# Later sums for the down product's last operands, and six attention pairs in other slots

## The chip, the core and the metric

The kernel runs on one core of a Trainium2 chip. The engines that compute are TensorE (PE), VectorE (DVE), ScalarE (ACT) and GpSimd (POOL); SyncE (SP) issues nearly all the DMAs. They run their own instruction streams and meet at semaphores. The metric is the device time of the one launch in microseconds.

## What is computed

Attention over keys and values that are averaged in groups of eight, and behind it two feed-forward layers over the 4608 resulting rows (the attention output with heads side by side), cut to its core:

```python
k_p = k.reshape(B, H, Sp, pool, D).mean(axis=3)      # B, H, S, D = 8, 8, 576, 64; pool = 8
v_p = v.reshape(B, H, Sp, pool, D).mean(axis=3)
scores = scale * np.matmul(q, k_p.transpose(0, 1, 3, 2))
attn = np.exp(scores - scores.max(-1)); attn = attn / (attn.sum(-1) + 1e-09)
x = np.matmul(attn, v_p)                             # as rows of 512
...
h = x @ w_in;  r = np.maximum(h, 0.0);  x = (s * (r * r) + b) @ w_out      # 512 -> 2048 -> 512
...
h = x @ w_in2; g = h * (1.0 / (1.0 + np.exp(-h)));  return g @ w_out2
```

## The kernel before, in words

**Units and phases.** The first 576 rows are worked in a first stage with plain products. The other 4032 rows form six units, two halves each: the widths of a half are `HALVES = (288, 288, 360, 360, 360, 360)`. The first two are the narrow units, the other four the wide ones. A unit has two phases, an even one for the first layer and an odd one for the second; there are twelve, `ph` 0 to 11. A phase has 56 slots, one granule of weights each (a row of `w_dram`, 512 KB, in a ring of six places), and 12 matmuls of 288 or 360 columns. Slots 0 to 27 are the up product, in four groups `g` of seven products `j` (a Strassen-like scheme: seven products of sums of quadrants in place of eight). Slots 28 to 55 are the down product; its slot `d` is 0 to 27, its operands stand in `DOWN` as (product j, half h), two slots each, so operand `idx` is used in d = 2 idx and 2 idx + 1: (0,0), (1,0), (0,1), (1,1), (2,0), (2,1), (3,0), (3,1), (4,0), (4,1), (5,0), (5,1), (6,0), (6,1).

**How an operand is made.** Every operand is a quadrant of the hidden layer `gq` or a difference of two. `combine(ph, j, h)` on DVE writes the difference in place (L1269), ACT writes the rounded high part (`dhi`, into `sp_hi`), DVE the rest (`dlo`, L1282 in even phases for some operands, L1285 otherwise, into `sp_lo`), in the loop `down_slot`, with `dhi` and `dlo` of operand idx + 3 in slot d = 2 idx + 1. `combined` counts the sums in the order of `COMBOS`. `form` adds a product that has ended in PSUM to its quadrant (L1244, L1246).

**x of the next unit.** In odd phases, `load_x` on SP brings the next unit's input from `xa_dram` (L512) into the last quadrant of `gq`, which must be free by then: it waits for `dlo` of operand 7. SP reaches it in its slot 28 + RING + 10, between two ring loads, and `load_gran` for slot n waits until PE has done slot n - 6. SP works in order, so what stands behind a waiting instruction waits too. DVE and ACT make x's operands from it in the slots `XR_SLOTS` of the odd phase (`x_slot`: xlo, L1290, and xsum, L1306); in even phases they make those of the second layer from `yb` near the end.

**Attention.** 32 pairs of heads, one `t` each, are spread over the slots by a table written by hand: `UNIT_TURNS` has for each unit the base slots of its pairs and the offsets of 13 turns, `TURN_NAMES`: scores, sub, exp, sum, norm, turn0, lo0, turn1, lo1, values0, add0, values1, add1. A unit's slots count from 0 to 111 over both phases. scores, turn0/1 (transposes) and values0/1 are PE's (L650, L664, L677); sub, sum, norm, lo0/1 and add0/1 are DVE's (L1147, L1152 to L1157, L1160, L1166, L1172); exp and the copies are ACT's; POOL averages keys and values. All of a slot's attention turns stand on each engine ahead of the slot's other work. All use one PSUM tile `t_ps`: turn0 waits for norm, turn1 for lo0, values1 for add0, the scores of the next pair for add1. `sub` of a pair writes `probs`, whose storage holds the last pair's output, so it waits until that has been stored to `xa_dram`; SP issues the store in the slot of add1 plus 7.

## Time and profile before

| | before |
|---|---|
| median of 3 runs | 1683.53 us (1678.99 to 1684.2) |
| profiled execution | 1683.26 us, span 1681.5 us |
| PE busy | 1601.1 us, 95% |
| DVE, ACT, POOL busy | 62%, 54%, 14% |
| mean granted clock of PE | 0.985 |
| DMA | 483.82 MB, 288 GB/s on average |
| chain that ended last | PE 73%, DVE 10%, DMA 9%, ACT 4% |

The span runs from the first to the last instruction; the device time is 1.8 us longer. A busy share says how full an engine is over the whole, not what holds the kernel in a stage: for that one reads a stretch at a time, and in it which wait of PE ends last, who ended it, and what that engine did before.

### The profile page before, as it was taken

To read this page: it belongs to the slowest core of one execution; us is meant where nothing else is said; L and a number is where in the kernel's file an instruction comes from. 1 tells how busy PE (TensorE), PEld (TensorE's weight loads), DVE (VectorE), ACT (ScalarE), POOL (GpSimd) and SP (SyncE) were. 2 spreads that over 40 slices of the span, in tenths; PEclk is the share of its full clock that TensorE was granted. 3 is DMA by queue.
4 is the path that set the end of the run, shared out by engine and by line. 5 is a ranking of instruction groups with operands and counts; after the bars stand their busy time and mean duration, and the time that the engine had idled before them with its cause. 6 is when DMAs were issued, how large, how long until landed. Compare 5 with 4: busy or idle time off the path is not lost.

```text
span 1681.5 us, 26389 instructions
## 1 busy us (share of the span) xinstructions
PE 1601.1 (95%) x10582; PEld 1583.9 (94%) x10582; DVE 1049.7 (62%) x1201; ACT 904.7 (54%) x1156; POOL 237.5 (14%) x294
## 2 busy tenths in 40 slices
PE   7999998888899889899999999999999999999998
PEld 6999897888899879899999999999999999999998
DVE  6787785565574664664765855756747656537454
ACT  4675654634545535547545557455466455474442
POOL 5310120121120221211201101102012010000000
PEclk9999999999999999999999999999999999999999
DMA  5899898887989878898888998888888888988886
GB/s 194 309 347 359 342 372 335 291 261 262 299 304 337 288 255 275 267 355 273 281 262 262 311 304 264 274 269 270 309 295 277 264 262 260 336 267 270 265 266 219
DMA packets 138008, 483.82 MB, mean 288 GB/s; under 512 B 14752, under 2 KB 14752, under 8 KB 135840
## 3 DMA queue, kind: packets, MB, share of 16 engines
q1 hardware_dynamic: 134080, 472.70, 83.0%
q10 hardware_dynamic: 3808, 9.44, 1.4%
q8 instruction: 85, 1.39, 0.3%
q14 instruction: 35, 0.29, 0.1%
HBM read 405.67 MB, written 76.41 MB: 287 GB/s over the span
## 4 chain that ended last, share of the span: by engine, by line
PE 73%; DVE 10%; DMA 9%; ACT 4%; issue 3%; SPq 0%; DVEq 0%; ACTq 0%
PE a_ps L806 19%; PE a_ps L784 18%; PE b_ps L806 14%; PE b_ps L784 13%; DMA xa_dram<-probs 5%; PE a_ps L710 2%; DMA w_raw<-weights 2%; PE t_ps L664 2%; PE t_ps L677 2%; DMA ring<-w_dram 2%; DVE w_sum L1200 1%; DVE gq L1269 1%; PE t_ps L650 1%; DVE sp_lo L1285 1%; DVE probs L1147 1%
## 5 line engine op out<-in xcount | busy, mean ns | idle before, releaser
L784 PE MATMUL a_ps<-xc_hi,ring 128*128 128x360 f32 (+1 forms) x1536 | 390.1, 323 | 16.4 <-DVE gq L1244 8.3
L806 PE MATMUL a_ps<-sp_hi,ring 128*128 128x360 f32 (+1 forms) x1536 | 375.0, 323 | 5.3 <-DMA ring<-w_dram 5.3
L784 PE MATMUL b_ps<-xc_hi,ring 128*128 128x360 f32 (+1 forms) x1152 | 290.6, 318 | 4.2 <-DMA ring<-w_dram 1.8
L784 PEld LDWEIGHTS a_ps<-xc_hi,ring 128*128 128x128 f32 x1536 | 272.3, 191 | 19.4 <-DVE gq L1244 10.4
L806 PEld LDWEIGHTS a_ps<-sp_hi,ring 128*128 128x128 f32 x1536 | 273.1, 194 | 5.8 <-issue 5.7
L1285 DVE TENSOR_TENSOR sp_lo<-gq,sp_hi 128x1440 fp32r<-128x1440 f32 (+3 forms) x156 | 197.2, 1283 | 122.6 <-ACT sp_hi L979 122.4
L806 PE MATMUL b_ps<-sp_hi,ring 128*128 128x360 f32 (+1 forms) x1152 | 273.4, 316 | 0.0
L806 PE MATMUL a_ps<-sp_lo,ring 128*128 128x360 f32 (+1 forms) x768 | 247.3, 322 | 0.0
L784 PE MATMUL a_ps<-xc_lo,ring 128*128 128x360 f32 (+1 forms) x768 | 244.8, 319 | 0.0
L784 PEld LDWEIGHTS b_ps<-xc_hi,ring 128*128 128x128 f32 x1152 | 201.6, 188 | 6.2 <-ACT gq L1001 3.3
L806 PEld LDWEIGHTS b_ps<-sp_hi,ring 128*128 128x128 f32 x1152 | 198.6, 188 | 0.0
L979 ACT ACTIVATE sp_hi<-gq 128x1440 fp32r<-128x1440 f32 (+3 forms) x156 | 161.5, 1061 | 48.5 <-PE a_ps L806 36.0
L806 PE MATMUL b_ps<-sp_lo,ring 128*128 128x360 f32 (+1 forms) x576 | 182.0, 316 | 0.0
L784 PE MATMUL b_ps<-xc_lo,ring 128*128 128x360 f32 (+1 forms) x576 | 181.9, 316 | 0.0
L574 POOL TENSOR_TENSOR k_stage<-k_stage 128x288 f32<-128x288 f32 (+1 forms) x58 | 46.8, 808 | 862.6 <-DMA k_stage<-kT 860.3
L1269 DVE TENSOR_TENSOR gq<-gq 128x1440 f32<-128x1440 f32 (+3 forms) x120 | 160.5, 1346 | 2.5
L806 PEld LDWEIGHTS a_ps<-sp_lo,ring 128*128 128x128 f32 x768 | 148.8, 194 | 0.0
L784 PEld LDWEIGHTS a_ps<-xc_lo,ring 128*128 128x128 f32 x768 | 146.9, 191 | 0.0
L574 POOL TENSOR_TENSOR v_stage<-v_stage 72x512 f32<-72x512 f32 (+2 forms) x90 | 103.3, 1148 | 263.0 <-DMA v_stage<-vP 258.1
L1244 DVE TENSOR_TENSOR gq<-b_ps,gq 128x720 f32<-128x720 f32 (+1 forms) x96 | 81.9, 853 | 78.7 <-PE b_ps L784 78.6
L1282 DVE SCALAR_TENSOR_TENSOR sp_lo<-gq,b_sign,sp_hi 128x1440 fp32r<-128x1440 f32 (+3 forms) x60 | 80.3, 1344 | 63.4 <-ACT sp_hi L977 63.3
L784 PEld LDWEIGHTS b_ps<-xc_lo,ring 128*128 128x128 f32 x576 | 108.2, 188 | 0.0
(168 smaller groups left out, 2508.6 us busy)
## 6 DMA issues: line engine op xcount, KB each, us to landing
ring<-w_dram SPq DMA_DIRECT2D x672, 512.0 KB, 4.5
w_dram<-w_stage SPq DMA_DIRECT2D x32, 1024.0 KB, 5.8
w_dram<-ring SPq DMA_DIRECT2D x48, 512.0 KB, 5.5
w_raw<-weights SPq DMA_DIRECT2D x16, 1024.0 KB, 6.2
k_stage<-kT SPq DMA_DIRECT2D x30, 288.0 KB, 5.4
q_sb<-qT SPq DMA_DIRECT2D x30, 288.0 KB, 5.7
v_stage<-vP SPq DMA_DIRECT2D x30, 288.0 KB
xa_dram<-probs SPq DMA_DIRECT2D x28, 288.0 KB, 5.3
```

Source lines behind the costliest of these rows:

```text
L574: nc.gpsimd.tensor_tensor(left, left, right, ALU.add).then_inc(partial, 1)
L650: last = nc.tensor.matmul(bank_s[:, n, g * 2 * SP:(g + 1) * 2 * SP], buf["q"][:, j * P:(j + 1) * P], buf["kp"], start=True, stop=True)
L664: last = nc.tensor.transpose(bank[0:SP, j * P:(j + 1) * P], buf["probs"][:, g * SP:(g + 1) * SP], ident[:, :])
L677: last = nc.tensor.matmul(bank_v[:, n, 0:HB], buf["vp"][:, e * P:(e + 1) * P], buf[pt][:, cols], start=(pt == "pT_hi"), stop=(pt == "pT_lo"))
L710: last = nc.tensor.matmul(bank[:, half, 0:HB], w, xc_of(x, HB)[:, b, k, :], start=(not end and k == 0 and m == 0), stop=(end and k == 1 an ...
L784: last = nc.tensor.matmul(bank[:, half, 0:th], w, xc_of(x, th)[:, j, k, :], start=(first and k == 0 and i == 0), stop=(k == 1 and i == 2), ...
L806: last = nc.tensor.matmul(bank[:, m, 0:th], w, split_of(g, th, turn, 2 * c + half), start=(first and half == 0 and i == 0), stop=(end and ...
L979: nc.scalar.activation(dst, src, ACT.Copy).then_inc(dhi_ready, 1)
L1244: nc.vector.tensor_tensor(part, acc(bank, th), part, ALU.add).then_inc(quad_formed, 1)
L1269: nc.vector.tensor_tensor(dst, left, right, ALU.subtract).then_inc(combined, 1)
L1282: nc.vector.scalar_tensor_tensor(out=dst, in0=src, scalar=b_sign[:, 0:1], in1=hi, op0=ALU.add, op1=ALU.subtract).then_inc(dlo_ready, 1)
L1285: nc.vector.tensor_tensor(dst, src, hi, ALU.subtract).then_inc(dlo_ready, 1)
```

## The change

Three things move. First, the sums for the operands of products 4 and 6 of the down product are made later: in d = 7, 9, 13 and 17, where they were made in d = 3, 5, 7 and 9. Second, what hangs on this: `load_x` waits in addition for the last sum that reads the last quadrant, (4, 1), and stands two slots later on SP; the first slots for x's operands move from 15, 17, 19, 21, 23 to 17, 19, 20, 22, 23. Third, the six pairs of each narrow unit have other base slots: 1, 16, 31, 46, 64 and 79 in place of 2, 17, 32, 47, 62 and 77. The fourth has a table of its own, with no turn from the offset 7 to 9, that is in the last three slots of the even phase: its scores to turn0 are in slots 46 to 52 and the rest begins with lo0 in slot 56, the first of the odd phase. It had turn0 in 53, lo0 in 54, turn1 in 55. Everything computed stays the same, with the same number of instructions on each engine.

```diff
+LATE_COMBOS = {7: (4, 0), 9: (4, 1), 13: (6, 0), 17: (6, 1)}
 XCOMBOS = (1, 4, 2, 6)
-XR_SLOTS = (15, 17, 19, 21, 23, 25, 27)
+XR_SLOTS = (17, 19, 20, 22, 23, 25, 27)
...
-SIX = tuple((2 + 15 * n, TIGHT) for n in range(6))
+OVER_X = (0, 1, 2, 3, 4, 6, 10, 11, 12, 14, 15, 16, 17)
+SIX = ((1, TIGHT), (16, TIGHT), (31, TIGHT), (46, OVER_X), (64, TIGHT), (79, TIGHT))
...
                     sp.wait_ge(dlo_ready, (2 * s - 1) * SPLITS + PIECE_END[7])
+                    sp.wait_ge(combined, (2 * s - 1) * len(COMBOS) + COMBOS.index((4, 1, 0)) + 1)
...
-                    if layer and slot == SLOTS_UP + RING + 10 and s + 1 < UNITS:
+                    if layer and slot == SLOTS_UP + RING + 12 and s + 1 < UNITS:
                         load_x(s + 1)
...
-                if d in (3, 5):
-                    combine(ph, 4, idx - 1)
-                elif d in (7, 9):
-                    combine(ph, 6, idx - 3)
+                if d in LATE_COMBOS:
+                    combine(ph, *LATE_COMBOS[d])
```

`TIGHT` is (0, 1, 2, 3, 4, 6, 7, 8, 9, 11, 12, 13, 14), as before. Below, lines of after are up to four higher than those of before for the same operation.

DVE, fourth phase (the second narrow odd one), from slot 33 on. L1285 is dlo, L1269 a combine, L1172 add0 and add1, L1244 form, L1290 xlo. Before:

```order
L1285 TENSOR_TENSOR sp_lo<-gq,sp_hi 128x1152
L1269 TENSOR_TENSOR gq<-gq 128x1152
L1172 TENSOR_TENSOR probs<-t_ps,probs 64x576
L1285 TENSOR_TENSOR sp_lo<-gq,sp_hi 128x1152
L1269 TENSOR_TENSOR gq<-gq 128x1152
L1285 TENSOR_TENSOR sp_lo<-gq,sp_hi 128x1152
L1269 TENSOR_TENSOR gq<-gq 128x1152
L1285 TENSOR_TENSOR sp_lo<-gq,sp_hi 128x1152 x2
L1244 TENSOR_TENSOR yb<-b_ps,yb 128x2x288
L1285 TENSOR_TENSOR sp_lo<-gq,sp_hi 128x1152
L1290 TENSOR_TENSOR xc_lo<-gq,xc_hi 128x720
```

The same engine and place after, from slot 33 on, where L1289 is dlo, L1273 a combine, L1176 add0 and add1, L1248 form:

```order
L1289 TENSOR_TENSOR sp_lo<-gq,sp_hi 128x1152
L1176 TENSOR_TENSOR probs<-t_ps,probs 64x576
L1289 TENSOR_TENSOR sp_lo<-gq,sp_hi 128x1152
L1273 TENSOR_TENSOR gq<-gq 128x1152
L1176 TENSOR_TENSOR probs<-t_ps,probs 64x576
L1289 TENSOR_TENSOR sp_lo<-gq,sp_hi 128x1152
L1273 TENSOR_TENSOR gq<-gq 128x1152
L1289 TENSOR_TENSOR sp_lo<-gq,sp_hi 128x1152 x2
L1273 TENSOR_TENSOR gq<-gq 128x1152
L1248 TENSOR_TENSOR yb<-b_ps,yb 128x2x288
L1289 TENSOR_TENSOR sp_lo<-gq,sp_hi 128x1152 x2
```

Before, the three combines in it are (4, 1), (6, 0) and (6, 1), with (4, 0) just above; after, they are (4, 0), (4, 1) and (6, 0), and (6, 1) follows. Combine (4, 1), for which the load of x waits now, stands where (6, 1) stood, and add0 and add1 are two slots later.

SP, the same phase, with what each row waits for: the store of a pair's output (L517), the ring loads (L505) and the load of x (L512). Before:

```order
L466 DMA v_stage<-vP 72x1024 [waits v_used]
L505 DMA ring<-w_dram 128x1024 [waits gran_done] x3
L517 DMA xa_dram<-probs 128x576 [waits x_summed]
L505 DMA ring<-w_dram 128x1024 [waits gran_done] x2
L512 DMA gq<-xa_dram 128x4x720 [waits x_stored,dlo_ready]
L505 DMA ring<-w_dram 128x1024 [waits gran_done] x25
```

After, the same place on SP:

```order
L469 DMA v_stage<-vP 72x1024 [waits v_used]
L508 DMA ring<-w_dram 128x1024 [waits gran_done] x3
L521 DMA xa_dram<-probs 128x576 [waits x_summed]
L508 DMA ring<-w_dram 128x1024 [waits gran_done] x2
L516 DMA gq<-xa_dram 128x4x720 [waits x_stored,combined,dlo_ready]
L508 DMA ring<-w_dram 128x1024 [waits gran_done] x23
```

The store and the load of x keep their distance; both come two ring loads later, so that the first ring load behind x is that of slot 46 where it was that of slot 44.

DVE at the edge from the third phase to the fourth (L1290 and L1306 are xlo and xsum from `yb`, L1166 is lo0 and then lo1). Before:

```order
L1306 TENSOR_TENSOR yb<-yb 128x2x288
L1290 TENSOR_TENSOR xc_lo<-yb,xc_hi 128x576 x2
L1166 TENSOR_TENSOR pT_lo<-t_ps,pT_hi 72x576
L1290 TENSOR_TENSOR xc_lo<-yb,xc_hi 128x576
L1306 TENSOR_TENSOR yb<-yb 128x2x288
```

After, at the same edge, L1294 and L1310 are xlo and xsum, L1170 is lo0 and then lo1:

```order
L1310 TENSOR_TENSOR yb<-yb 128x2x288
L1294 TENSOR_TENSOR xc_lo<-yb,xc_hi 128x576 x3
L1310 TENSOR_TENSOR yb<-yb 128x2x288
L1170 TENSOR_TENSOR pT_lo<-t_ps,pT_hi 72x576
L1294 TENSOR_TENSOR xc_lo<-yb,xc_hi 128x576
L1170 TENSOR_TENSOR pT_lo<-t_ps,pT_hi 72x576
```

lo0 of the fourth pair moves from before xlo(5) and xsum(6) to behind them.

## Rows read from the trace of the kernel before

**Rows 1.** Busy time by stretch: third, fourth and sixth phase, with columns' names.

```profile
core 0: us, PE busy (x) PEld busy (x) DVE busy (x) ACT busy (x) POOL busy (x), PEclk, DMA share, GB/s
...
510.60:635.30 124.70, 109.89 (x779) 107.53 (x778) 72.94 (x96) 64.79 (x91) 23.22 (x31) 0.94 0.83 285
635.30:746.00 110.70, 103.00 (x738) 100.64 (x738) 70.70 (x84) 57.12 (x76) 24.19 (x23) 0.96 0.88 300
...
863.70:982.70 119.00, 117.81 (x730) 117.00 (x729) 77.04 (x82) 61.03 (x72) 15.40 (x18) 1.00 0.85 284
```

**Rows 2.** Waits of PE: us in total, times, longest us.

```profile
PE t_ps L664 <- DVE pT_lo L1166: 12.9, 5, 3.6
PE t_ps L664 <- DVE probs L1160: 12.1, 7, 4.3
...
PE a_ps L806 <- DMA ring<-w_dram: 5.3, 2, 3.0
```

**Rows 3.** The chain that ended last, ends of the narrow odd phases: start, us, what.

```profile
489.74 8.13 PE a_ps L806 x48
...
504.24 6.37 PE a_ps L806 x48
...
725.09 8.13 PE a_ps L806 x48
```

**Rows 4.** Busy time in the 7 us behind three waits of PE.

```profile
571.33:578.33 7.00, 7.00 (x53) 7.00 (x54) 6.83 (x6) 1.91 (x2) 2.80 (x2) 1.00 0.92 250
589.90:596.90 7.00, 7.00 (x35) 6.86 (x36) 3.20 (x3) 1.04 (x2) 0.00 (x0) 0.58 0.27 91
695.46:702.46 7.00, 6.83 (x42) 6.50 (x43) 4.33 (x5) 2.97 (x4) 3.71 (x4) 0.81 0.62 205
```

**Rows 5.** Timeline of PE: start, us, instruction, [idle before it <- releaser].

```profile
571.33 0.40 PE L677 MATMUL t_ps<-pT_hi,vp 72*128 72x288 f32 x1 [1.53 <-DVE probs L1172]
...
589.90 1.28 PE L664 MATMUL t_ps<-ident,probs 128*72 128x128 f32 x5 [3.81 <-DVE probs L1160]
...
631.08 1.28 PE L664 MATMUL t_ps<-ident,probs 128*72 128x128 f32 x5 [3.59 <-DVE pT_lo L1166]
...
695.46 1.28 PE L664 MATMUL t_ps<-ident,probs 128*72 128x128 f32 x5 [2.63 <-DVE pT_lo L1166]
```

**Rows 6.** Timeline of SP around the load of x, second and fourth phase.

```profile
480.49 0.55 SPq L512 DMA_DIRECT2D gq<-xa_dram  x1
...
711.92 1.68 SPq L505 DMA_DIRECT2D ring<-w_dram  x2
717.39 0.54 SPq L512 DMA_DIRECT2D gq<-xa_dram  x1
```

**Rows 7.** Timeline of DVE, third and fourth phase.

```profile
548.74 0.97 DVE L1147 TENSOR_TENSOR probs<-t_ps,rowmax 128x432 f32<-128x432 f32 x2 [2.36 <-DMA xa_dram<-probs]
...
570.53 0.74 DVE L1172 TENSOR_TENSOR probs<-t_ps,probs 64x576 f32<-64x576 f32 x1
...
583.86 1.35 DVE L1269 TENSOR_TENSOR gq<-gq 128x1152 f32<-128x1152 f32 x1
...
588.94 0.90 DVE L1160 TENSOR_TENSOR probs<-probs,rden 128x720 f32<-128x720 f32 x1
...
636.76 0.76 DVE L1290 TENSOR_TENSOR xc_lo<-yb,xc_hi 128x576 fp32r<-128x576 f32 x1 [5.74 <-ACT xc_hi L992]
...
638.11 0.75 DVE L1166 TENSOR_TENSOR pT_lo<-t_ps,pT_hi 72x576 fp32r<-72x576 f32 x1
...
711.84 1.36 DVE L1285 TENSOR_TENSOR sp_lo<-gq,sp_hi 128x1152 fp32r<-128x1152 f32 x1 [0.31 <-ACT sp_hi L979]
713.11 2.45 DVE L1269 TENSOR_TENSOR gq<-gq 128x1152 f32<-128x1152 f32 x1
715.48 1.88 DVE L1285 TENSOR_TENSOR sp_lo<-gq,sp_hi 128x1152 fp32r<-128x1152 f32 x1
```

**Rows 8.** Waits of SP's queue for the load of x.

```profile
SPq L512 <- DVE sp_lo L1285: 11.1, 5, 2.9
```

**Rows 9.** Timeline of POOL at the same place in the fourth phase.

```profile
712.14 4.00 POOL L574 TENSOR_TENSOR v_stage<-v_stage 72x512 f32<-72x512 f32 x2 [7.18 <-DMA v_stage<-vP]
```

**Rows 10.** DMA issues of the page: xcount, KB each, median us to landing.

```profile
xa_dram<-probs SPq DMA_DIRECT2D x28, 288.0 KB, 5.3
```

## The prediction

> **What bounds the kernel now.** Names: a unit's even phase is its slots a0 to a55, its odd phase b0 to b55; slots 28 to 55 are the down product. I read first the table by stretch [rows 1]. A narrow even phase has 124.70 us with TensorE (PE) busy for 109.89, a narrow odd one 110.70 with 103.00, and a wide odd one 119.00 with 117.81. The granted clock is 0.94 and 0.96 in the narrow ones and 1.00 in the wide. So only the two narrow units hold idle PE to be won; a wide phase has about 1 us. The waits of PE [rows 2] name two causes: pT_lo and probs of the attention, both made by VectorE (DVE), and twice a ring granule from DMA, 5.3 us together, 3.0 the longer.
>
> **What a lost microsecond costs.** At full clock 48 matmuls, four granules, take 6.37 us, so a granule is 1.59 us; behind the two DMA waits the same 48 take 8.13, which is 1.76 more each [rows 3]. In 7 us behind a wait of 3.81 us the granted clock is 0.58, so 0.42 x 7 = 2.9 us are lost; behind 2.63 it is 0.81, 1.3 us; behind one of up to 1.5 us it is 1.00 [rows 4, 5]. The two levels are 2.4 and 1.2 GHz. I price a drop at 1.8 us behind waits of 2.3 to 3 us, at 2.8 behind longer ones, at nothing up to 1.6; between 1.6 and 2.3 no row tells, and both ends stay open.
>
> **Part 1: the load of x.** In the narrow odd phases SP issues the next unit's x at 480.49 and 717.39. SP had reached it when b37 was done, at 713.3 (the last ring load in front of it ends at 713.60) [rows 6]. It then waited for dlo of the second half of product 3, DVE's L1285 that starts at 715.48 and takes 1.88, so until 717.36 [rows 7]. The ring loads of b44 and b45 stood behind it. SP's waits show this five times, 11.1 us in all, 2.9 the longest [rows 8]. PE resumes at 489.74 and 725.09 [rows 3], 9.25 and 7.70 us after the issue of x. Price now: 3.0 + 1.76 = 4.8 us and 2.3 (5.3 less 3.0) + 1.76 = 4.1 us.
>
> After: SP reaches x two slots later, when b39 is done, and waits for combine(4, 1). On DVE dlo(6) starts at 711.84, 1.4 before b37's end. From there DVE has dlo(6) 1.27 (start to start, 711.84 to 713.11), combine(4, 0) 1.27, add1 0.7 (now here), dlo(7) 1.27 and combine(4, 1) 1.27: 5.8 us. values1 now stands in b36, which puts b37's end 0.5 later. So x can go 3.9 us after b37, and b39 is 3.2 after it: 0.7 us late. The rows also show DVE stretched beside POOL, a combine of 2.45 where another takes 1.35, with POOL in its adds of v [rows 7, 9]; v lands two slots later too, so one combine may be stretched again, and x goes 1.8 late. I take 1.8. The granule of b46 waits for b40 anyhow, 1.6 after b39. Its data come 7.7 to 9.25 after x, so 9.5 to 11.05 after b39; PE wants them 6 granules after b39, at 9.57. What is left is 0 and 1.5 us, with no drop: **gain 4.1 + 3.3 = 7.4 us**. Ends: 8.9 if both waits go, 0 if combine(4, 1) is another 2.3 us late. In the wide phases x has the same order, a slot is 1.97 us and PE has no such wait: nothing.
>
> On the stretched combine, the Trainium skill (SBUF — State Buffer, section "SBUF: two separate sides") says that DVE operations with two inputs from SBUF and GpSimd's operations take turns under an exclusive lock on a shared port pair. The 2.45 and 1.88 beside POOL agree. By that rule the collision moves with v and is not removed, which is the 1.8; without it x goes 0.7 late and the gain would be 1.1 more, 8.5.
>
> **Part 2: attention and sums in the narrow even phases.** Now, per unit: 124.70 - 109.89 = 14.8 us idle [rows 1] plus drops of 1.8, 2.8 and 2.8 behind the waits at a20 (2.3), a38 (3.81) and a55 (3.59) [rows 5]: 22.2 us. At a20 form(2, 1) stands behind sub, which waits for the store of x (DVE at 548.74, 2.36 idle). At a38 PE waits for norm (588.94), in front of which DVE ran a chain with combine(4, 1) at 583.86 [rows 7]; combine(4, 0) and (6, 0) stood in it too.
>
> After, place by place. (i) a19: add1, store and sub all move by one slot and form(2, 0) stands now behind sub: 2.3 + 1.8, as before. (ii) a29: values1 needs add0, which on DVE stands behind dlo(2, 1) and two combines and ends at 571.27 (570.53 + 0.74) [rows 7]. That chain hangs on granule a26 and on ScalarE, where the copy of values0 now comes ahead of it (0.6 us, eating most of the 0.9 that PE is ahead by then). So add0 ends where it did and PE arrives a slot (1.6) and 0.9 earlier: 1.5 + 1.6 + 0.8 = 3.9, + 2.8. (iii) a37: norm has dlo(4) and dlo(5) ahead of it but none of the three combines. sub starts when the store lands, about 6 us behind a30 (the page's median is 5.3 from issue [rows 10]); then 0.9 + 1.3 + 1.3 + 0.8 bring norm to within 0.3 of PE's arrival. The wait of 3.81 is gone. (iv) a39: late next is lo0. dlo(6), combine(4, 0), dlo(7), combine(4, 1) and lo0 take 4 x 1.27 + 0.75 = 5.9 behind norm, PE has 0.5 + 2 x 1.59 of work: 2.2 to 2.5, + 1.8. (v) a44 and a46: add0 and add1 now stand ahead of form and dlo: nothing. (vi) a52: sub in a47 waits for the store issued when a45 is done, 5.3 us; then 0.9 + 0.75 + 1.27 + 0.75 + 1.3 + 1.35 + 0.9 lead to the end of norm, 12.5 behind a45; PE, with scores of 1.2, arrives at 6 x 1.59 + 1.2 = 10.8: 1.7, no drop. (vii) b1 in place of a55: turn1 needs lo0, which now stands behind xlo(5) and xsum(6), and these behind ScalarE's copy of the last bank. The same three run now from 636.76 to 638.86 [rows 7], 3.6 behind a55's end; PE has one granule: 2.0. Sum: 4.1 + 6.7 + 0.3 + 4.3 + 1.7 + 2.0 = 19.1, and 1.8 more if the last drops the clock. **Gain 3.1 us, or 1.3; I take 3.0 per unit.**
>
> **Part 3: the narrow odd phases, without x.** Now: 7.7 us idle [rows 1] and drops of 1.8 and 1.3, less b44's 4.1, is 6.7; the largest piece is turn1 at b29, 2.63 [rows 5]. The ends of matmuls are modelled, and some ten short waits cost PE about 0.25 more each than they show: 9.2. After: sub at b9 waits for the store with form(1, 0) and form(1, 1) behind it, 1.6 in two pieces; sub at b24 holds form(3, 0), 6.3 + 1.6 behind b22 against 6.0 for PE: 1.9; exp then stands behind first_op(3, 0) on ScalarE: 0.9 at b29; turn1 at b31 waits for lo0 behind dlo(2, 1), three combines and two dlo: 3.1 + 2.3. Sum 9.8, or 11.6 with a drop at b26. **A loss: 1.2 taken per unit, 0.6 to 2.4.**
>
> **Part 4: XR_SLOTS.** From b45 DVE has some 17 us of work in 11 slots of 1.59 = 17.5, in wide phases 20 in 21.7. The last xlo is needed only about 3 us into the next phase, which is the cover: nothing. Were it gone, each us of it would be a us of PE.
>
> **Sum.** 7.4 + 2 x (3.0 - 1.2) = 11.0 us. The profiled execution took 1683.26 (span 1681.5), the median of the three runs is 1683.53, 0.3 above. 1683.5 - 11.0 = **1672.5 us**. By its own ends: gain 8.9 + 2 x (3.1 + 0.9 - 0.6) = 15.7, and 5.5 + 2 x (1.3 - 2.4) = 3.3: 1668 to 1680.
>
> **The rivals.** (A) *The x load still holds the ring.* DVE comes to combine(4, 1) 2.3 us later than I counted, by a second stretched operation and a late add1. For it: two operations were stretched there (2.45, 1.88). Against: two combines fewer stand ahead. Gain only 3.6: 1680. (B) *Only x wins.* The waits of attention move and cost a little more than before, at a29 and b31 above all: 7.4 less 2: 1678. (C) *Slower.* The place is sub, which now stands ahead of form and dlo in a47, b9 and b24 and waits for the store of x. If stores land 2.2 us later than I took, a52 becomes 3.9 + 2.8, b26 4.1 + 2.8, b12 1.8 more and a19 1.3 more: some 12 us per unit, 24 in all, and the kernel takes 1696. For it: at a20 even now sub waits 2.36 for a store. The point from which it loses is about 1 us above my landing times, where half of that eats the 11. (D) *Larger gain.* Stores land within 5 us throughout and DVE reaches its sums earlier, so that neither a29 nor a39 drops the clock: 2 x (2.8 + 1.8 + 1.5) more: 1660.
>
> **Chances.** Forecast 0.50, A 0.13, B 0.14, C 0.13, D 0.10. A measurement of this kernel tells 0.3%, 5 us, from no change; faster is below 1678.5. The forecast gives 0.46 faster and 0.04 same, A 0.13 same, B 0.12 faster and 0.02 same, C slower, D faster: 0.68, 0.19, 0.13. The range reaches from inside D to beyond A, 1663 to 1683; C and part of D are left out.
>
> **What the profile would show.** Part 1: SP's wait at the load of x under 2 us in the narrow phases, and no PE wait of over 2 us for the ring in b46. Part 2: no wait for probs above 1 us at a37; one of 3 to 4 us for probs at a29; waits for pT_lo at a39 and b1, where a55 has none. Part 3: turn1 at b31 waits 3 us. I would be wrong if PE still waits for norm at a37, or if the wide phases change by more than 0.5 us each.

## The result and the profile after

The changed kernel takes **1688.64 us**, the median of 20 runs (1680.5 to 1692.43), against 1680.56 us for the kernel before (20 runs, 1672.94 to 1686.91). The ratio is **1.0041**, with a 95% interval of 1.0026 to 1.0055. It is slower by 0.4%, where 11 us less were forecast. The profiled execution of after took 1685.94 us (span 1684.2), 2.7 below its median; that of before stood 2.7 above the median of its 20 runs. So the two profiles show only 2.7 us of the 8.1 between the medians, and what follows from them is the account of one execution each.

The same three stretches as in [rows 1], each from the end of a phase's predecessor to its own end, in the profile after:

```profile
513.70:633.90 120.20, 107.07 (x773) 104.95 (x772) 73.28 (x95) 64.55 (x89) 20.12 (x28) 0.96 0.84 288
633.90:748.40 114.50, 102.78 (x744) 100.49 (x743) 71.03 (x85) 58.11 (x77) 21.39 (x27) 0.97 0.87 297
...
866.70:985.60 118.90, 117.61 (x728) 116.81 (x728) 77.39 (x82) 60.63 (x72) 14.75 (x18) 1.00 0.86 279
```

The narrow even phase went from 124.70 to 120.20 us, the narrow odd one from 110.70 to 114.50, the wide one stayed. The other narrow pair did less well: the first phase went from 132.78 to 132.95, the second from 110.48 to 112.12. Both odd phases lost, 1.6 and 3.8 us. Part of these moves is only the edge: the wait of 3.59 us at a55 stood in the even phase, and the one at b1 that came for it stands in the odd phase.

The waits of PE, as in [rows 2]:

```profile
PE t_ps L668 <- DVE pT_lo L1170: 15.0, 7, 3.1
PE b_ps L788 <- DVE gq L1248: 10.9, 7, 2.8
PE t_ps L668 <- DVE probs L1164: 8.7, 7, 2.4
PE t_ps L681 <- DVE probs L1176: 8.5, 3, 3.8
PE a_ps L788 <- DVE gq L1248: 5.3, 8, 0.9
...
PE a_ps L810 <- DMA ring<-w_dram: 3.5, 2, 2.1
```

The wait for norm (L1164) fell from 12.1 to 8.7 and that for the ring from 5.3 to 3.5. The wait for lo0 (L1170) rose from 12.9 to 15.0. And there is a line that [rows 2] don't have: PE waits for `form` (L1248) in b_ps, 10.9 us in seven waits. In before the two lines on `form` had 8.3 us for a_ps and 1.3 for b_ps, 9.6 together, where after has 16.2. These are the two of the kernel before:

```profile
PE a_ps L784 <- DVE gq L1244: 8.3, 6, 3.4
PE b_ps L784 <- DVE gq L1244: 1.3, 3, 0.6
```

Now the places, in the timeline of PE, third and fourth phase; the number in brackets is the idle time, as in [rows 5]:

```profile
550.91 0.40 PE L788 MATMUL b_ps<-xc_hi,ring 128*128 128x288 f32 x1 [1.81 <-DVE gq L1248]
572.60 0.61 PE L681 MATMUL t_ps<-pT_hi,vp 72*128 72x288 f32 x1 [3.81 <-DVE probs L1176]
580.14 1.46 PE L654 MATMUL t_ps<-kp,q_sb 128*128 128x144 f32 x10 [1.27 <-DVE probs L1176]
...
592.03 0.74 PE L668 MATMUL t_ps<-ident,probs 128*72 128x128 f32 x5 [0.86 <-DVE probs L1164]
598.04 1.17 PE L668 MATMUL t_ps<-ident,probs 128*72 128x128 f32 x5 [2.08 <-DVE pT_lo L1170]
...
626.79 0.74 PE L668 MATMUL t_ps<-ident,probs 128*72 128x128 f32 x5 [2.36 <-DVE probs L1164]
637.58 0.74 PE L668 MATMUL t_ps<-ident,probs 128*72 128x128 f32 x5 [2.08 <-DVE pT_lo L1170]
...
701.15 1.28 PE L668 MATMUL t_ps<-ident,probs 128*72 128x128 f32 x5 [3.08 <-DVE pT_lo L1170]
730.70 0.37 PE L810 MATMUL a_ps<-sp_hi,ring 128*128 128x288 f32 x1 [2.14 <-DMA ring<-w_dram]
```

These are the slots a19, a29, a31, a37, a39, a52, b1, b31 and b46. What stands behind a52 is in the timeline of DVE. `sub` (L1151) waits 3.19 us for the store of the last pair, and `form` (L1250), `dlo` (L1289) and the rest of the chain to norm (L1164) stand behind it:

```profile
619.80 0.97 DVE L1151 TENSOR_TENSOR probs<-t_ps,rowmax 128x432 f32<-128x432 f32 x2 [3.19 <-DMA xa_dram<-probs]
620.69 0.81 DVE L1250 SCALAR_TENSOR_TENSOR yb<-a_ps,sign,yb 128x576 f32<-128x576 f32 x1
621.42 1.34 DVE L1289 TENSOR_TENSOR sp_lo<-gq,sp_hi 128x1152 fp32r<-128x1152 f32 x1
...
625.83 0.90 DVE L1164 TENSOR_TENSOR probs<-probs,rden 128x720 f32<-128x720 f32 x1
```

**The load of x.** In the second phase combine(4, 1) starts at 486.02 and takes 1.89; x goes when it ends, and PE takes up b46 9.5 us later, at 497.48, after a wait of 1.39. In the fourth phase, in the timeline of DVE:

```profile
718.20 2.44 DVE L1273 TENSOR_TENSOR gq<-gq 128x1152 f32<-128x1152 f32 x1
```

The timeline of SP in both phases, as in [rows 6]:

```profile
487.97 0.54 SPq L516 DMA_DIRECT2D gq<-xa_dram  x1
...
717.69 1.65 SPq L508 DMA_DIRECT2D ring<-w_dram  x2
721.88 0.54 SPq L516 DMA_DIRECT2D gq<-xa_dram  x1
```

Here combine(4, 1) ended at 720.64, stretched to 2.44 beside POOL, as counted. But x went only at 721.88, 1.24 us later: it waited for something else. SP's waits from 700 to 730 name it:

```profile
SPq L515 <- DMA xa_dram<-probs: 2.5, 1, 2.5
```

It is the store of pair 19, the last pair whose output is in that x; `load_x` waits for `x_stored` too. The same stretch of the kernel **before** has these two rows, and the prediction did not read them:

```profile
SPq L511 <- DMA xa_dram<-probs: 3.2, 1, 3.2
SPq L512 <- DVE sp_lo L1285: 0.5, 1, 0.5
```

In before, of the 3.8 us that SP stood at x in the fourth phase, 3.2 were for the store and 0.5 for dlo. The prediction put it all down to dlo, because dlo came last.

### The profile page after: what moved, and what is told of

The parts are those of the page before. It is cut to its first block, busy times and chain, and to the rows that moved or that the text cites. A ratio compares the mean times of both kernels' runs of the same rounds, so it can differ in the third digit from the quotient of the medians.

```text
span 1684.2 us, 26389 instructions
## 1 busy us (share of the span) xinstructions
PE 1606.0 (95%) x10582; PEld 1589.8 (94%) x10582; DVE 1048.1 (62%) x1201; ACT 904.4 (54%) x1156; POOL 220.4 (13%) x294
## 3 DMA queue, kind: packets, MB, share of 16 engines
q8 instruction: 85, 1.39, 0.3%
## 4 chain that ended last, share of the span: by engine, by line
PE 76%; DVE 9%; DMA 8%; ACT 4%; issue 3%; SPq 0%; DVEq 0%; ACTq 0%
PE a_ps L810 19%; PE a_ps L788 18%; PE b_ps L810 13%; PE b_ps L788 12%; DMA xa_dram<-probs 5%; PE a_ps L714 3%; PE a_ps L738 2%; PE t_ps L668 2%; PE t_ps L681 2%; DMA ring<-w_dram 2%; DVE gq L1273 1%; PE b_ps L714 1%; DVE sp_lo L1289 1%; PE t_ps L654 1%; PE t_ps L738 1%
## 5 line engine op out<-in xcount | busy, mean ns | idle before, releaser
L788 PE MATMUL b_ps<-xc_hi,ring 128*128 128x360 f32 (+1 forms) x1152 | 293.4, 320 | 13.0 <-DVE gq L1248 10.9
L1289 DVE TENSOR_TENSOR sp_lo<-gq,sp_hi 128x1440 fp32r<-128x1440 f32 (+3 forms) x156 | 199.9, 1302 | 137.5 <-ACT sp_hi L983 137.1
L810 PE MATMUL b_ps<-sp_hi,ring 128*128 128x360 f32 (+1 forms) x1152 | 277.7, 319 | 0.0
L788 PEld LDWEIGHTS b_ps<-xc_hi,ring 128*128 128x128 f32 x1152 | 203.6, 190 | 15.0 <-DVE gq L1248 12.7
L810 PEld LDWEIGHTS b_ps<-sp_hi,ring 128*128 128x128 f32 x1152 | 202.1, 191 | 0.1
L1273 DVE TENSOR_TENSOR gq<-gq 128x1440 f32<-128x1440 f32 (+3 forms) x120 | 154.9, 1299 | 2.5
L578 POOL TENSOR_TENSOR k_stage<-k_stage 128x288 f32<-128x288 f32 (+1 forms) x58 | 42.0, 724 | 856.9 <-DMA k_stage<-kT 854.6
L578 POOL TENSOR_TENSOR v_stage<-v_stage 72x512 f32<-72x512 f32 (+2 forms) x90 | 99.3, 1103 | 289.8 <-DMA v_stage<-vP 284.9
L1248 DVE TENSOR_TENSOR gq<-b_ps,gq 128x720 f32<-128x720 f32 (+1 forms) x96 | 81.8, 852 | 79.1 <-PE b_ps L788 79.1
L810 PEld LDWEIGHTS b_ps<-sp_lo,ring 128*128 128x128 f32 x576 | 110.1, 191 | 0.0
```

Of the source, the lines that this page charges most:

```text
L578: nc.gpsimd.tensor_tensor(left, left, right, ALU.add).then_inc(partial, 1)
L788: last = nc.tensor.matmul(bank[:, half, 0:th], w, xc_of(x, th)[:, j, k, :], start=(first and k == 0 and i == 0), stop=(k == 1 and i == 2), ...
L810: last = nc.tensor.matmul(bank[:, m, 0:th], w, split_of(g, th, turn, 2 * c + half), start=(first and half == 0 and i == 0), stop=(end and ...
L1248: nc.vector.tensor_tensor(part, acc(bank, th), part, ALU.add).then_inc(quad_formed, 1)
L1273: nc.vector.tensor_tensor(dst, left, right, ALU.subtract).then_inc(combined, 1)
L1289: nc.vector.tensor_tensor(dst, src, hi, ALU.subtract).then_inc(dlo_ready, 1)
```

## The experiments

All ratios are to the kernel before, with 95% intervals, measured beside it on the same chip. They come from four such series on different chips, so the difference of two ratios carries the intervals of both. x late means the place of `load_x` two slots later on SP, and the slots of x's operands that go with it.

**The change taken apart, first cut.** Late sums and late x with the old base slots (`SIX` as before):

```diff
-SIX = ((1, TIGHT), (16, TIGHT), (31, TIGHT), (46, OVER_X), (64, TIGHT), (79, TIGHT))
+SIX = tuple((2 + 15 * n, TIGHT) for n in range(6))
```

> The late sums, the later load of x and the later slots for x's operands alone; all attention pairs in the slots of before. Theory S (the new attention slots are what costs; the late sums pay): three combines fewer stand ahead of norm at a38, so its wait of 3.8 us falls under 1.5 and its drop of the clock goes, and the wait for the ring in the odd phases moves from b44 to b46 and shrinks: 6 to 12 us faster than before. Theory X (the late sums cost: combine(4, 1) holds SP's queue and the ring load of b46 waits as long as that of b44 did): the wait at b46 is 2.5 us or more with a drop in both odd phases, and the time is within 3 us of before or above it.

Measured: 1.0014 (0.9996 to 1.0032), 3 us slower where theory S had 6 to 12 faster. As theory X had it, the wait for the ring stayed long, though with 2.02 us one of the two is under its 2.5. The other half, the kernel before with the new `SIX` and nothing else:

> The new slots of the six pairs alone; sums, load of x and its operands as before. Theory S: 8 to 14 us slower than before, with waits of about 4 us at a29, 2 to 4 us at a37 and a39 (all four early combines stand ahead of norm and lo0 again), 2 us at b1, 2 us at b26 and 3 us at b31. Theory X: the slots are neutral, within 3 us of before.

Measured: 1.0104 (1.0077 to 1.0131), 1698.17 us. The new slots by themselves lose more than the whole change, and more than the 8 to 14 us of theory S. Two cuts of them, again on the kernel before, the first three pairs of a unit moved and the last two:

```diff
-SIX = tuple((2 + 15 * n, TIGHT) for n in range(6))
+SIX = ((1, TIGHT), (16, TIGHT), (31, TIGHT), (47, TIGHT), (62, TIGHT), (77, TIGHT))
...
+SIX = ((2, TIGHT), (17, TIGHT), (32, TIGHT), (47, TIGHT), (64, TIGHT), (79, TIGHT))
```

> Only the first three pairs of each narrow unit one slot earlier (bases 1, 16, 31), the others in the slots of before, sums as before. Theory S, by place: a30's wait of 1.5 us becomes one of 3.8 with a drop at a29, 2 x (2.3 + 2.8) = 10 us of loss; the wait for norm at a38 moves to a37 and falls by what PE came later, about 4 us per unit; in all 0 to 6 us slower. Theory X: within 3 us.

> Only the two pairs in the odd phases two slots later (bases 64, 79), all else as before. Theory S, from the rows of the odd phases: new waits of 0.8 and 0.7 us at b12 and b13, 2.2 at b26 for 1.5 at b25, 0.6 at b29 and 3.1 at b31 for 2.6 at b29: 2 to 5 us slower in all. Theory X: within 2 us.

Measured: 1.0052 (1.0032 to 1.0073) and 1.0043 (1.0027 to 1.0060). That is 9.9 and 7.6 us between the medians, where at most 6 and 5 had been expected. Together 0.95%, of the 1.04% of all six. So both groups lose, and for the fourth pair, over the edge of the phases, nothing is left that the intervals could tell from zero. In last2_only a good part is at the load of x, which the expectation did not name: the store of pair 19 lands at 718.40, x goes at 718.47, and PE's wait for the ring in the fourth phase is 4.36 us where it was 2.28.

**The load of x alone.** The kernel before with

```diff
-                    if layer and slot == SLOTS_UP + RING + 10 and s + 1 < UNITS:
+                    if layer and slot == SLOTS_UP + RING + 12 and s + 1 < UNITS:
-XR_SLOTS = (15, 17, 19, 21, 23, 25, 27)
+XR_SLOTS = (17, 19, 20, 22, 23, 25, 27)
```

> Part 1 alone: the kernel before with load_x two slots later on SP and the first slots of x's operands moved as in the change; sums and pairs of attention as before. SP should find the load of x free at once (dlo of operand 7 is 1.5 to 4 us old when b39 is done), so x goes at b39's end. Theory 1 (what counts is the delay behind SP's held queue): x goes 1.5 us earlier than in the kernel after, which waits for combine(4, 1), PE comes to b46 9.6 after b39 and finds the granule there: the waits 3.0 and 2.3 with their drops go, 6 to 8 us less, ratio 0.995 to 0.996. Theory 2 (what counts is the bytes of x ahead of the ring load, which take 9 to 10 us from x's issue to the next granule): the wait goes from 3.0 and 2.3 to about 0.5 to 1 without a drop, which gives the same ratio, within 0.1%. If x needs more than 10.5 us to let the next granule through, it is 1 us or more with a drop in one of the two phases: ratio 0.997 to 0.998. The two first come apart by the wait at b46: 0 or 0.5 to 1.

Measured: **0.9962** (0.9943 to 0.9980), 6.4 us less. SP finds x free in the second phase and almost so in the fourth, and PE's wait is 1.20 in the fourth and 0.67 in the second, with no drop of the clock. Theory 2 had 0.5 to 1, theory 1 nothing. SP's timeline, and below it PE's, in before with x late:

```profile
480.96 0.55 SPq L512 DMA_DIRECT2D gq<-xa_dram  x1
...
711.72 0.54 SPq L512 DMA_DIRECT2D gq<-xa_dram  x1
```

```profile
722.03 0.37 PE L806 MATMUL a_ps<-sp_hi,ring 128*128 128x288 f32 x1 [1.20 <-DMA ring<-w_dram]
```

From the issue to PE's next granule it takes 10.3 us here, where 7.70 and 9.25 were read before. So even an x that goes at once leaves about 1 us of wait. The store of pair 19 had landed at 711.34, with b39 done at 711.28: it is just in time. With the new slots the pair itself is two slots later, and so is its store; the two slots that x was given are then used up.

**What the bytes of x do.** The kernel after, with a quarter of x's columns loaded for the later units (the rest of x is left out):

```diff
-                sp.dma_start(rows_of(x_of(2 * s), HALVES[s]), xa_dram[:, :, start_of(s):start_of(s) + 2 * HALVES[s]]
+                n = 2 * HALVES[s] // (4 if s else 1)
+                sp.dma_start(rows_of(x_of(2 * s), HALVES[s])[:, :, 0:n], xa_dram[:, :, start_of(s):start_of(s) + n]
```

> The changed kernel with only a quarter of the columns of x loaded for units 1 to 5, at the same place and with the same waits (the rest of x is left out, so the result is not the reference's). Theory B (the bytes of x in front of the ring loads make b46 wait, not SP's wait for the sum): the waits of 1.4 and 2.1 us at b46 go, 2 to 6 us faster than the changed kernel. Theory Q (SP's queue, held until combine(4, 1), makes it wait): the waits stay within 0.5 us of what they were.

Measured: 1.0011 (0.9993 to 1.0028), 5 us under the ratio of the change. There is no wait at b46 any more, though x goes 1.7 and 3.3 us behind b39, no earlier than in the change (1.4 and 2.9). It is the bytes ahead of the granule that PE waits for. So the load in two halves, with one ring load between them, nothing left out:

```diff
+                ks = slice(2 * part, 2 * part + 2)
+                sp.dma_start(rows_of(x_of(2 * s), HALVES[s])[:, ks, :],
+                             xa_dram[:, ks, start_of(s):start_of(s) + 2 * HALVES[s]]).then_inc(x_landed, DMA)
...
+                    if layer and slot == SLOTS_UP + RING + 13 and s + 1 < UNITS:
+                        load_x_part(s + 1, 1)
```

> The kernel after with the load of x in two halves, the second behind the next ring load (one granule later on SP). Everything is still loaded. If the bytes of x in front of the granule of b46 are what makes it late (with a quarter of the columns there was no wait at all), the wait at b46 (1.4 and 2.1) goes to under 0.6, b47's wait stays under 0.6, and the kernel takes 3 to 5 us less than the one after: ratio 1.0015. If it is the load's fixed cost, or the slower transfer from this layout, two loads cost more than one: b46 stays at 1.4 to 2.1 or b47 takes over with 1 to 2: 1.003 to 1.006. x lands one granule later, which the operands of x in slots 45 and 46 may feel: ACT then waits up to 1.5 us in them, off PE's path.

Measured: 1.0025 (1.0005 to 1.0045). The wait at b46 is gone in the second phase and 0.78 us in the fourth, where b47 has another of 1.16. Together that is 1.9 us for the 2.14 of before the split, without the drop of the clock. The gain over the change is 0.16%, with intervals that overlap, so it is not shown in the time.

**The wait for the store.** `probs` holds the last pair's output, so `sub` waits until it is stored. A buffer of its own for the output takes that wait away from `sub`; the copy of values0, eight slots later, waits instead:

```diff
-        x_stage = probs[:, 0:S]
+        x_stage = sb("x_own", [P, S])[:, :]
...
-                    if t > PAIRS:
-                        dve.wait_ge(x_stored, (t - PAIRS) * DMA)
...
+                    if e == 0 and t > PAIRS:
+                        act.wait_ge(x_stored, (t - PAIRS) * DMA)
```

> The kernel before, with a buffer of its own for a pair's output, so that sub no longer waits for the store (the copy of the next pair's values0 does). Theory St (the store in front of sub is what makes form late at a20 and ScalarE late at b25): the waits of 2.3 to 3.4 us at a20 and of 1.3 to 1.5 at b25 go, norm at a38 comes 1 to 2 us earlier; 6 to 14 us faster than before. Theory D (DVE is simply full there, the store is hidden): the waits stay above 1.5 us and the time is within 3 us.

> The changed kernel with the same own buffer. Theory St: the waits at a19, b12, b13, b26 and most of a52 go, 12 to 20 us faster than the changed kernel, so about 1670 to 1678; what stays is a29 (3.8 us), b1 (2.1) and b31 (3.1). Theory D: within 3 us of the changed kernel, about 1688.

Measured: before with the buffer 0.9911 (0.9884 to 0.9938), after with it 0.9886 (0.9863 to 0.9910). Both won more than expected, 16.6 us for 6 to 14 and about 26 for 12 to 20. The change costs 0.4% with the shared buffer and nothing that the intervals could show with its own. In after with the buffer PE's wait for `form` in b_ps has fallen from 10.9 to 2.1 us, and `sub` at a52 runs as soon as rowmax is there, norm with it, so that PE doesn't wait at a52. A line of PE's waits, and below it DVE's timeline at a52, both of after with its own buffer:

```profile
PE b_ps L788 <- DVE gq L1248: 2.1, 4, 0.9
```

```profile
606.90 0.97 DVE L1140 TENSOR_REDUCE rowmax<-t_ps 128x6 f32<-128x432 f32 x2
607.91 0.97 DVE L1151 TENSOR_TENSOR probs<-t_ps,rowmax 128x432 f32<-128x432 f32 x2
608.80 0.81 DVE L1250 SCALAR_TENSOR_TENSOR yb<-a_ps,sign,yb 128x576 f32<-128x576 f32 x1
...
613.94 0.91 DVE L1164 TENSOR_TENSOR probs<-probs,rden 128x720 f32<-128x720 f32 x1
```

**The square.** Four more kernels fill the table of sums, slots and buffer, with x late in all of them:

> The fourth corner: late sums and late load of x with the old base slots of the pairs, and the own buffer, so that sub never waits for the store. The other corners are 0.991 (old slots, old sums) and 0.989 (new slots, new sums). If the store alone makes the new slots lose (slots only took 1.010 of the time of before), this takes the same as the kernel after with the buffer, 0.987 to 0.990. If the slots bring something by themselves once the store is out of the way, as a38 (3.0) and a55 (3.6) stand in the old slots and not in the new ones, it is slower than that by 0.3% or more: 0.992 to 0.994.

> The change without its late sums: new base slots of the pairs, load of x two slots later without the wait for combine(4, 1). New slots without the late load took 1.0104, the late load alone 0.9962. If the parts add, this takes 1.0066 and the late sums then gain 0.25% in the new slots (1.0041), where in the old ones they lose 0.5% (from 0.9962 to 1.0014). If the late sums cost as much in the new slots as in the old ones, this takes 0.999. Waits by place: a37 2.7 and b26 2.6 to 2.9 as with the slots alone, b46 at most 1.2 where the slots alone had 3.1 and 3.9 at b44.

> Old sums, old slots, load of x late, own buffer for a pair's output. The buffer alone took 0.9911, x late alone 0.9962. If they add: 0.9873, 1660 us for a kernel before of 1682; then the late sums (sums_own: 0.9881) bring nothing even without the store's wait. If the buffer has already taken what x wins (the store of a pair stands in front of x on SP, and its landing too), 0.990 to 0.991. Waits: a38 3.0, a55 3.6 and b29 2.5 stay, b46 0 to 1.2.

> Old sums, new slots, x late, own buffer. If the new slots lose only through the wait for the store, this equals xlate_own within 0.2% (0.987 to 0.989). If the new slots need the late sums too (norm at a37 and form at b26 stand behind the early sums on DVE, 2.7 and 2.6 to 2.9 in the slots alone), it is 0.3% or more above xlate_own and above after_own (0.9886): 0.991 to 0.994.

| x late | old slots | new slots |
|---|---|---|
| shared buffer, old sums | 0.9962 (0.9943 to 0.9980) | 1.0074 (1.0050 to 1.0098) |
| shared buffer, late sums | 1.0014 (0.9996 to 1.0032) | 1.0041 (1.0026 to 1.0055), the change |
| own buffer, old sums | 0.9872 (0.9853 to 0.9891) | 0.9930 (0.9903 to 0.9956) |
| own buffer, late sums | 0.9881 (0.9844 to 0.9918) | 0.9886 (0.9863 to 0.9910) |

Three things follow. The **new slots** cost 1.12% with the old sums and the shared buffer, and 0.58% with the own one, each to within about 0.3%: roughly half of it is the store in front of `sub`. My theory after the first runs, that it was all of it, fell with slots_xlate_own. With late sums and the own buffer the slots cost only 0.05% (to within 0.4%), which points to norm and add1 behind the early sums on DVE for the other half. A part of both is again the store in front of x: the waits at b46 in the fourth phase are 2.43 and 2.53 in the new slots, with either buffer, and 1.20 and 1.15 in the old ones. In slots_xlate PE waits at a37, b36 and b46 (timeline of PE, third and fourth phase):

```profile
598.07 0.74 PE L665 MATMUL t_ps<-ident,probs 128*72 128x128 f32 x5 [2.13 <-DVE probs L1161]
...
718.20 0.41 PE L678 MATMUL t_ps<-pT_hi,vp 72*128 72x288 f32 x1 [1.39 <-DVE probs L1173]
737.37 0.37 PE L807 MATMUL a_ps<-sp_hi,ring 128*128 128x288 f32 x1 [2.43 <-DMA ring<-w_dram]
```

In after the first of them is 0.86 (592.03 above) and the second is no longer among the waits over 0.6. So the **late sums** belong to the new slots, where they win 0.3% (0.4% with the own buffer); the intervals just touch in both cases. In the old slots they lose 0.5% with the shared buffer: combine(4, 1) ends 2.5 us behind b39, and the waits at b46 are 2.02 and 3.08 in place of at most 1.20, both with a drop of the clock; a47 goes from 1.17 to 2.45. And the **late x** is the only part of the change that wins by itself.

**The order on DVE at the start of the down product.** combine(2, 0) in d = 0 in place of slot 27, first on the kernel before, then on after with the own buffer, then on before with the own buffer and x late:

```diff
-                    combine(ph, 2, 0)
...
+                if d == 0:
+                    combine(ph, 2, 0)
```

> The kernel before, with the one sum combine(2, 0) moved on DVE from slot 27 to slot 28, behind that slot's attention. Theory C (add0 in the even and lo0 in the odd phase are late because this chain of dlo and sums stands ahead of them, 1.3 us each): a30's wait falls from 1.5 to about 0.3 us, b29's from 2.6 to about 1.3 and loses its drop of the clock: 4 to 8 us faster. Theory D (other work fills the gap): within 3 us.

> The kernel after with the own buffer for a pair's output, and in addition the sum combine(2, 0) on DVE one slot later (in d = 0, where it stood with combine(1, 1) in slot 27). Before, the same move took 1.2 us off the wait at b29 and its drop of the clock. Here the wait nearest to it is a31 (1.54 and 1.97 with the own buffer) in the even phases and b31 (3.08) in the odd ones; combine(2, 0) stands ahead of the chain that both hang on only if DVE has no idle time between slot 28 and slot 31. If the order on DVE is what holds PE in these slots, a31 goes to under 1 and the kernel takes 1658 to 1662. If DVE has idle time there (it waits for granule 30's operand or for the attention's copies), nothing changes: 1663, ratio 0.988 to 0.989.

> xlate_own with combine(2, 0) one slot later, which took 1.2 us and the clock's drop off the wait at b29 in the kernel before (0.9970). If the three parts add: 0.9843, 1655 us, the fastest of all. If the chance drops of the clock and the a38 and a55 waits decide, it is within 0.2% of xlate_own: 0.9855 to 0.989. Waits: b29 1.4 in place of 2.5, the others as in xlate_own.

Measured: 0.9970 (0.9949 to 0.9991), 0.9868 (0.9834 to 0.9903) and **0.9862** (0.9842 to 0.9883). The first took the wait at b29 from 2.53 and 2.63 to 1.36 in both phases, and with it the one drop that stood behind the 2.63, but left a30 at 1.52 and 1.69, where 0.3 had been expected. In the second, a29 went from 3.81 to 2.56 and a31 rose from 1.54 and 1.97 to 2.08 and 2.23: PE waits for the same add1 a little later, where under 1 had been expected, and the time tells nothing, as its interval overlaps that of after_own. The last is the fastest kernel of all, 1656.21 us against 1679.77 for before beside it, but it stands above the 0.9843 at which the parts would add up, and its interval overlaps that of xlate_own.

## Why the prediction was wrong

The sum was 7.4 + 2 x (3.0 - 1.2) = 11.0 us less; it came out 8.1 more. Two steps failed: the gain of 3.0 us per unit in the even phases (part 2), which did not come, and x going only 1.8 us late (part 1), which left out the store that x waits for. By parts, as the ratios measured them one on top of the other: the load of x -0.38%, the slots on top of it +1.12%, the late sums on top of both -0.33%. The prediction had -0.44% for the first and -0.21% for the other two, which were +0.79%, 13 us. (The sum's own low end took 5.5 for the first part, while the working gives 0 as its end, and its high end has a 0.9 that stands nowhere in the working.)

**Part 1, the load of x: right in mechanism and, alone, in size; a cover was missed in the whole.** Alone it won 6.4 us, 3.4 to 9.6 by its interval, for 7.4. In the change, the two waits that were priced at 4.8 and 4.1 us became 1.39, and 2.14 with a drop. In the 7 us behind the latter the granted clock is 0.76, the fourth row here:

```profile
598.04:605.04 7.00, 7.00 (x41) 6.76 (x41) 1.24 (x1) 3.50 (x4) 1.84 (x4) 0.76 0.57 196
637.58:644.58 7.00, 7.00 (x54) 7.00 (x55) 2.18 (x3) 4.44 (x6) 0.00 (x0) 1.00 0.71 241
626.79:633.79 7.00, 7.00 (x54) 7.00 (x55) 5.85 (x8) 3.28 (x5) 0.49 (x1) 1.00 0.69 239
730.70:737.70 7.00, 7.00 (x41) 7.00 (x42) 2.36 (x4) 1.15 (x2) 0.00 (x0) 0.76 1.00 380
```

0.24 x 7 = 1.7 us. So 5.2 us are left and 3.7 are won, for 7.4. The step that failed is "x goes 1.8 late": in the second phase it went 1.4 late (487.97, b39 done at 486.55) and the wait left is the 1.5 of the forecast, in the fourth it went 2.87 (721.88, b39 at 719.01). combine(4, 1) ended 1.6 behind b39, within the count on DVE; the store of pair 19 landed 1.2 after that. It had been the longer of SP's two waits even before, covered by 0.5 us of dlo, and the sentence that the store and x keep their distance in the order should have been a warning: what keeps its distance wins nothing by moving. The time from x's issue to the next granule was 9.5 and 8.8 us, the first 0.25 above the 7.7 to 9.25 of the prediction.

**Part 2, the even phases: most places right, but no gain.** Forecast and measured (third phase) waits in us: a19 2.3 and 1.81; a29 3.9 and 3.81; a37 0.3 and 0.86; a39 2.2 to 2.5 and 2.08; a52 1.7 and 2.36; b1 2.0 and 2.08. a31, 1.27, was not in the list at all: the next pair's scores wait for add1, which follows add0 from a29. So the sum of waits was 12.4 to 12.7, and is 14.3, and a42 has another 0.85 behind lo1. Part of a52 is the store again: it landed late enough for `sub` to wait 3.19. In the first unit the waits are much the same, 14.4 (a19 2.81, a29 3.81, a31 0.69, a37 0.87, a39 2.08, a52 2.04, b1 2.09).

What a slot takes over 1.59 us and the work of its turn is its loss, waits and clock together. Counted so, without a3 to a5 where the ring still fills (8.2 us before, 9.1 after), the even phases hold 22.7 us in both units before, for the 22.2 of the prediction. After, with b1, they hold 25.0 in the first unit and 21.4 in the second, 23.2 on average, for its 19.1. So the second unit, the one that the prediction read, gained 1.3, its low end, and the first lost 2.3: half a microsecond is lost per unit where 3.0 were to be gained. The two units differ by 3.6 us with the same waits. The difference is the clock: behind a19 and a52 it drops in the first unit and not in the second, and the prediction had priced a drop at a19 and none at a52.

**Part 3, the odd phases: right in the profile.** The same count gives 9.2 before, as forecast, and 10.6 after, for 9.8 to 11.6. The waits were named: b26 2.22 and 2.19, b31 3.09 and 3.08. The time of the two pairs alone, 7.6 us more in last2_only, says that their move costs more than the 2.4 of the forecast; a part of what the forecast lacked is the store of pair 19 in front of x, at b44 there.

**Part 4 and the wide phases: right in sum.** The eight wide phases took 931.0 us before and 931.3 after. Single ones moved by up to 1.0 us, over the 0.5 that the prediction had set as its limit, and the moves cancel. Of its other signs in the profile, a29, a37, a39, b1 and b31 came as named; the wait in b46, to be under 2 us, was 2.14.

Of the shortfall of 19.1 us this explains 11.3: 3.7 in x, 7.0 in the even phases, 0.6 in the odd ones. Another 2.1 lie outside the parts: a3 to a5 lost 0.9, and the first phase began 1.2 us later (268.41 for 267.20), for a reason that stays open. The other 5.4 us are the distance of the two profiles from their medians, 2.7 each. Which of the places they are in is not shown.

**The price of a drop was no rule but a chance.** I had priced none behind waits up to 1.6 and took one as sure behind 2.3 to 3. Two of the four rows above follow waits of the same 2.08 us (a39 and b1); one has the clock at 0.76, the other at 1.00. The third follows 2.36 us and has 1.00. Counted over 18 traces of this study, PE's waits from 330 to 760 us, with the time at the lower level in the 7 us behind them (half of that is lost):

```
wait, us     waits  with a drop  mean us at half clock
1.4 to 1.7      27            6                    0.8
1.7 to 2.0      17            8                    1.6
2.0 to 2.2      37           18                    1.6
2.2 to 2.5      29           12                    1.4
2.5 to 2.8      41           26                    2.1
2.8 to 3.2      25           18                    3.1
3.2 to 5        47           46                    4.4
```

So a wait of 1.7 to 2.5 us costs 0.7 to 0.8 on top of itself on average, one of 2.5 to 2.8 costs 1.1, one of 2.8 to 3.2 costs 1.5, one above costs 2.2. The change has many in the middle: the sure drop of a38 is gone, but a29 has one now, and a39, a52, b1 and b26 are waits of about 2 us, each with about half a chance. That makes a single profile a poor witness. The executions bear this out: of the 23 of the kernel before that ran beside before_own, the fastest took 1675.18 us at a mean granted clock of 0.992, the slowest 1689.65 at 0.981.

**The rivals.** A, that x still holds the ring: its price, a gain of only 3.6 in place of 7.4, is what came (3.7), but by the store, not by a second stretched operation. B, that only x wins: the ratio of x alone (0.9962) is right for the half that it names, but attention costs not a little but 0.8%. C, the slower case, had 0.13. It named the right place, `sub` ahead of form and dlo, but not by its condition, stores that land 1 us later than taken. These are the times from issue to landing of the stores of pairs' outputs from 300 to 760 us, first before, then after:

```profile
DMA to landing us min/median/max: 3.6/5.6/7.1
DMA to landing us min/median/max: 4.1/5.4/6.6
```

The forecast had 5.3. The waits of `sub` did not grow either, as DVE's waits in the same stretch show, before and after:

```profile
DVE probs L1147 <- DMA xa_dram<-probs: 25.3, 8, 4.5
DVE probs L1151 <- DMA xa_dram<-probs: 20.3, 10, 3.8
```

What grew is their price. The own buffer is worth 0.89% to the kernel before and 1.55% to the one after, a difference of 0.66%, 11 us, which the intervals leave between about 5 and 18. So a store at its usual time, with form, dlo and norm behind the `sub` that waits for it, was enough, together with a31, with the store in front of x, and with drops at half chance. D was wrong: a29 and a39 both wait as counted.

The Trainium skill, in DMA: Bandwidth & Descriptors, section "Anatomy of one DMA — SWDGE (gpsimd) path", says that a DMA's end is late because the last write must be confirmed, above all in HBM, and gives about 2.0 us plus the bytes over 436 GB/s; for a store of 288 KB that is an estimate of 2.7 us by the Trainium skill, for DMAs that another engine issues. SP's stores here landed after 4.1 to 6.6 us in the narrow units, with the DMA engines 84 and 87% busy in the third and fourth phase. The measurement decides: by the Trainium skill's figure, an estimate again, six of the ten waits of `sub` in these units would be gone and the other four at most 1.0 us.

## What to carry to other kernels

A wait for several semaphores hides all but the last; before moving an instruction with such a wait, ask for each of them when it would be satisfied, and move what feeds it too. An operation that waits for a DMA's landing should not stand in front of the work of others on an in-order engine: here 288 KB of on-chip memory for a buffer of its own were worth 0.9% in the kernel before and 1.5% in the one after, more than any of the orders tried. And when a change trades one long wait for several of middle length, price the clock by its chance at each length and take more than one profile.

## What was not expected of the hardware

The granted clock falls behind waits of 1.7 to 2.8 us in 64 of 124 cases, and behind waits over 3.2 us in 46 of 47. The shortest wait with a drop behind it is one of 1.52 us. The length of a wait does not tell which: twelve of the waits in the table are of this same 1.52 us, all for add0 and with no other wait in the 7 us ahead, and five of them have the drop.

A load of 1.2 to 1.5 MB in front of a granule of 512 KB held PE's next granule back until 7.7 to 10.3 us after the load's issue (7.70 and 9.25 in before, 9.5 and 8.8 in after, 9.3 and 10.3 in before with x late). With a quarter of its columns the wait was gone; with the load in two halves it was gone in one phase and in the other 0.78 and, a granule on, 1.16. The operations of DVE beside POOL's adds were stretched again where v had moved: the combine of 2.44 us at 718.20 runs beside POOL's two adds from 717.58 to 721.24, where the same combine takes 1.35 elsewhere.
